# A fused attention and two-layer chain: variances asked for at the normalisation, a new order of gates and loads in the first batch, output products opened in five banks, and two weights merged in three passes

## The reference

```python
kv  = einsum('bhsd,bhse->bhde', k, v);  o = einsum('bhsd,bhde->bhse', q, kv)
x   = o / sqrt(mean(o*o, -1) + 1e-6) * g_norm          # 8 heads of 64
# 4 experts, each a causal attention; the two with the larger gate logits count
q, k, v = x @ wq[e], x @ wk[e], x @ wv[e]
a   = softmax(q @ k.T / 8, causal);   ye = a @ v @ wo[e]
x2  = sum over the two chosen e of softmax weight * ye
# gated layer
h   = gelu(x2 @ w_in);  u, g = h[:, :512], h[:, 512:]
vn  = (g - mean(g)) / sqrt(var(g) + 1e-6) * g_ln
out = x2 + (u * (w_sg @ vn + b_sg)) @ w_out
```

## Time and profile before

| | us |
|---|---|
| median of 3 runs (lowest, highest) | 836.63 (836.17, 839.96) |
| profiled execution, whole | 838.38 |
| its span, first to last instruction | 836.6 |
| PE busy | 812.7 (97%) |
| DVE busy | 484.8 (58%) |
| ACT busy | 370.6 (44%) |
| POOL busy | 193.1 (23%) |

### The profile page before, as it was taken

One profiled execution on the slowest core, in us unless ns is written; L12 is line 12 of the kernel. 1 busy time (PEld: TensorE's weight loads), 2 busy tenths in 40 slices (PEclk: granted clock), 3 DMA queues, 4 the chain that ended last, 5 costly groups with the idle time before them and its releaser, 6 DMA issues.

```text
span 836.6 us, 16871 instructions
## 1 busy us (share of the span) xinstructions
PE 812.7 (97%) x6637; PEld 727.7 (87%) x6637; DVE 484.8 (58%) x1272; ACT 370.6 (44%) x841; POOL 193.1 (23%) x246
## 2 busy tenths in 40 slices
PE   7988999999999999999999999999999999998998
PEld 4787898988889898998989889898989989898896
DVE  1767744485545855478534874458553685548840
ACT  0665513474235632455234661456323563255521
POOL 1621224003320133102230023300332013310320
PEclk9999999999999999999999999999999999999999
DMA  9819005040140304130050400504014000100001
GB/s 268 232 47 220 19 6 122 2 115 1 27 94 2 114 1 78 50 94 22 1 107 14 116 1 16 111 2 114 2 33 89 2 2 1 45 26 2 1 1 63
DMA packets 117406, 47.29 MB, mean 57 GB/s; under 512 B 94352, under 2 KB 110736, under 8 KB 117328
## 3 DMA queue, kind: packets, MB, share of 16 engines
q1 hardware_dynamic: 117328, 46.21, 22.0%
HBM read 35.19 MB, written 9.44 MB: 53 GB/s over the span
## 4 chain that ended last, share of the span: by engine, by line
PE 84%; DVE 10%; ACT 2%; DMA 1%; issue 1%; POOL 0%; SPq 0%; DVEq 0%; ACTq 0%; POOLq 0%
PE w L1025 29%; PE t L1025 23%; PE t L1086 7%; PE w L1056 6%; PE t L1071 5%; PE t L1168 3%; PE t L1153 2%; PE t L1176 2%; PE w L1123 2%; PE w L1235 2%; PE w L1071 2%; DVE bn L839 2%; DVE staged L849 1%; DVE big L834 1%; DVE big L854 1%
## 5 line engine op out<-in xcount | busy, mean ns | idle before, releaser
L1025 PE MATMUL w<-wout_s,big 128*128 128x512 f32 x432 | 108.1, 399 | 1.5 <-DVE big L854 0.6
L1025 PE MATMUL t<-big,wqk_s 128*128 128x288 f32 x768 | 105.7, 296 | 2.3 <-DVE wsgT_s L909 2.3
L1025 PE MATMUL w<-wsgT_s,big 128*128 128x288 f32 x768 | 107.3, 295 | 0.0
L1025 PEld LDWEIGHTS t<-big,wqk_s 128*128 128x128 f32 x768 | 102.5, 188 | 2.7 <-issue 2.6
L1025 PEld LDWEIGHTS w<-wsgT_s,big 128*128 128x128 f32 x768 | 103.8, 189 | 0.0
L811 DVE CUSTOM_DVE_ANT_0 w<-w,causal 128x64 f32<-128x64 f32 (+4 forms) x160 | 74.9, 518 | 38.8 <-PE w L1056 38.1
L1025 PEld LDWEIGHTS w<-wout_s,big 128*128 128x128 f32 x432 | 79.6, 188 | 20.3 <-DVE big L854 3.2
L585 POOL TENSOR_TENSOR yT<-squares,yT 128x256 fp32r<-128x256 f32 (+1 forms) x32 | 22.3, 696 | 283.9 <-ACT yT L710 283.9
L724 ACT ACTIVATE big<-work 128x576 fp32r<-128x576 f32 x32 | 22.0, 686 | 111.5 <-POOL work L612 96.1
L980 DVE SCALAR_TENSOR_TENSOR work<-w,gln_c,bias_t 128x576 f32<-128x576 f32 x32 | 26.2, 818 | 71.7 <-PE w L1025 71.0
L1025 PE MATMUL t<-w_s,yT 128*128 128x512 f32 x240 | 63.2, 404 | 4.5 <-POOL yT L585 4.5
(11 more groups left out here) (122 smaller groups left out, 1418.7 us busy)
## 6 DMA issues: line engine op xcount, KB each, us to landing
kin<-in_k_dram SPq DMA_DIRECT2D x8, 1024.0 KB, 6.3
vin<-in_v_dram SPq DMA_DIRECT2D x8, 1024.0 KB, 9.4
out_dram<-work SPq DMA_DIRECT2D x32, 256.0 KB, 2.1
qin<-in_q_dram SPq DMA_DIRECT2D x112, 72.0 KB, 2.4
staged_win<-in_moe_w_in_dram SPq DMA_DIRECT2D x4, 512.0 KB, 5.3
vin<-in_moe_w_sg_dram SPq DMA_DIRECT2D x4, 288.0 KB, 3.9
kin<-in_k_dram SPq DMA_DIRECT2D x8, 128.0 KB, 2.9
vin<-in_v_dram SPq DMA_DIRECT2D x8, 128.0 KB, 6.6
```

What stands on the lines that cost most here:

```text
L1025: last = nc.tensor.matmul(o, stationary(hs, c), mv(hm, c), start=c == of[0] and p == 0, stop=c == of[-1] and p == len(PASSES) - 1)
```

## The change

1. In part -1 `w2` is made like every other product: `wo` turned and `w_in` are split into HI and LO (unit `win`, ScalarE and VectorE; for `woT` both parts by VectorE) and multiplied in three fp32r passes, pass by pass instead of chunk by chunk. The parts lie in `wsgT_s`, `wout_s` and `wo_s` until these get their own contents.
2. In batch 0 `ranks` stays, the last two `wsgT` units and `qk (0, 1)` come before `weights` and `scale 0`, and `wsgR` before `scale 1`; `qk (1, 1)` takes slot `t0` instead of `t1`.
3. k of batch 1 is loaded as soon as `w_out` is split, v after `wsgT 4` (which is also where GpSimd now clears `vin`), q after `wsgR`.
4. In every batch GpSimd's variance and power stand at `norm j` instead of `h j`, and ScalarE's `vhat` of tiles 3 and 4 after `u 1` and `u 2` instead of `u 0` and `u 1`.
5. In the last batch `scale 2` comes before `values 0`, and `out_y` of all five tiles comes before the first `out_g`, in slots w0, w1, t0, t1, t2.

```diff
-    FIRST = [("woT", 0), ("woT", 1), ("w2", 0), ("w2", 1)] + [("kv", c) for c in range(DC)]
-    FIRST += [("qT", 0), ("qT", 1), ("qT", 2), ("o", 0), ("qT", 3), ("o", 1), ("qT", 4), ("o", 2),
-              ("o", 3), ("w2", 2), ("x", 0), ("o", 4), ("x", 1), ("x", 2), ...
+    FIRST = [("woT", 0), ("woT", 1), ("win", 0), ("win", 1), ("w2", 0), ("w2", 1)] + [("kv", c) for c in range(DC)]
+    FIRST += [("qT", 0), ("qT", 1), ("qT", 2), ("o", 0), ("qT", 3), ("o", 1), ("qT", 4), ("win", 2), ("o", 2),
+              ("o", 3), ("w2", 2), ("x", 0), ("o", 4), ("win", 3), ("x", 1), ("x", 2), ...
...
-        plan += [("ranks", 0), ("g_exp", 0), ("weights", 0), ("qk", (0, 1)), ("scale", 0)] + late(("wsgT", 4))
-        plan += [("qk", (EP, 1)), ("scale", 1)] + late(("wsgR", 0)) + [("qk", (1, 1))] + late(("split", "wo"))
+        if first:
+            plan += [("ranks", 0), ("g_exp", 0), ("wsgT", 3), ("qk", (0, 1)), ("wsgT", 4), ("weights", 0), ("scale", 0), ("qk", (EP, 1)),
+                     ("wsgR", 0), ("qk", (1, 1)), ("scale", 1), ("split", "wo")]
...
-        plan += values(0) + [("scale", 2)] + ([] if last else KV)
+        plan += [("scale", 2)] + values(0) if last else values(0) + [("scale", 2)] + KV
...
-    VHAT_AFTER = {("gelu", 2): 0, ("gelu", 3): 1, ("gelu", 4): 2, ("u", 0): 3, ("u", 1): 4}
+    VHAT_AFTER = {("gelu", 2): 0, ("gelu", 3): 1, ("gelu", 4): 2, ("u", 1): 3, ("u", 2): 4}
...
-    PLAN[B - 1] = attention(False, True) + MLP + [x for x in MIX if x[0] != "turn"] + [x for x in MIXED if x[0] in ("out_y", "out_g")]
+    PLAN[B - 1] = attention(False, True) + MLP + [x for x in MIX if x[0] != "turn"]
+    PLAN[B - 1] += [("out_y", t) for t in range(NT)] + [("out_g", t) for t in range(NT)]
...
             sp.wait_ge(wout_lo, FC)
+            load_kv(1, "k")
+            u.wait_full(sp, 0, ("wsgT", NT - 1))
+            sp.wait_ge(vin_padded, 1)
+            load_kv(1, "v")
             u.wait_full(sp, 0, ("wsgR", 0))
-            sp.wait_ge(vin_padded, 1)
-            load_kv(1)
             load_q_blocks(1)
...
-                    elif kind == "h":
+                    elif kind == "norm":
 
                         pool.wait_ge(var_ready, count(part, NT, j + 1))
...
+                    elif kind == "win":
+                        dve.wait_ge(win_hi, j + 1)
+                        nc.vector.tensor_tensor(win_split[j][:, LO, :], win_st[j], as_f32(win_split[j][:, HI, :]),
+                                                ALU.subtract).then_inc(win_lo, 1)
...
+                        for p, (hs, hm) in enumerate(((HI, HI), (LO, HI), (HI, LO))):
+                            if p == 1:
+                                u.wait_drained(pe, part, ("woT", j // 2))
+                            if p == 2:
+                                pe.wait_ge(win_lo, j + 1)
+                            for c in range(EP):
+                                x = ps[u.slot(part, ("w2", c))]
+                                for h in range(2):
+                                    last = nc.tensor.matmul(x[:, FF * h:FF * (h + 1)], woT_split[:, hs, 256 * j + P * c:256 * j + P * (c + 1)],
+                                                            win_split[j][:, hm, FF * h:FF * (h + 1)], start=j == 0 and p == 0,
+                                                            stop=j == DC - 1 and p == 2)
```

More of the change, by code:

```diff
@@ L156, in moe_chain @@
     SLOT_FIRST = {**SLOT, ("v", 1): "t2", ("v", 2): "t0", ("v", 3): "t2", ("wsgT", 0): "t1", ("wsgT", 1): "t3", ("wsgT", 2): "t1",
-                  ("wsgT", 3): "t3", ("wsgT", 4): "t1", ("wsgR", 0): "t3", ("qk", (EP, 1)): "t2", ("qk", (1, 1)): "t1"}
+                  ("wsgT", 3): "t3", ("wsgT", 4): "t1", ("wsgR", 0): "t3", ("qk", (EP, 1)): "t2", ("qk", (1, 1)): "t0"}
     SLOT_LAST = {**SLOT, ("v", 4): "t3"}
@@ L195, in units @@
                     got.append((("y", j // 2), Y_SLOT[j // 2]))
-            elif kind in ("split", "double", "exp", "scale", "gelu", "wout", "w2e", "yhi", "turn", "T_copy", "y_mul", "ranks",
+            elif kind in ("split", "double", "exp", "scale", "gelu", "wout", "w2e", "yhi", "turn", "T_copy", "y_mul", "ranks", "win",
                           "g_exp", "weights", "norm"):
@@ L207, in units @@
                     got.append((("u", 0), WIDE[0]))
-            elif kind in ("u", "vs", "woT"):
+            elif kind in ("u", "vs"):
                 got.append(((kind, j), WIDE[j % 2]))
             elif kind == "out_y":
-                got.append((("out", j), WIDE[(j - first_out(part)) % 2]))
+                got.append((("out", j), (WIDE + NARROW)[j] if part == B - 1 else WIDE[(j - first_out(part)) % 2]))
             elif kind == "out_g":
@@ L317, in moe_chain @@
         w_hi = sem("w_hi")
+        win_hi = sem("win_hi")
+        win_lo = sem("win_lo")
+        woT_hi = sem("woT_hi")
         wqk_lo = [sem("wqk_lo_0"), sem("wqk_lo_1")]
@@ L379, in moe_chain @@
         win_st = [staged_win[:, r, c * 2 * FF:(c + 1) * 2 * FF] for r in range(2) for c in range(2)]
-        woT_st = [staged_win[:, r, 4 * FF + 256 * c:4 * FF + 256 * (c + 1)] for r in range(2) for c in range(2)]
+        win_split = [wsgT_s[:, :, :, :].rearrange("p s t n -> p s (t n)")[:, :, 2 * FF * c:2 * FF * (c + 1)] for c in range(2)]
+        win_split += [wout_s[:, :, :, :].rearrange("p s c n -> p s (c n)")[:, :, 2 * FF * c:2 * FF * (c + 1)] for c in range(2)]
+        woT_split = wo_s[:, :, :, :].rearrange("p s c n -> p s (c n)")
         wqk_st = staged_wqk[:, :].rearrange("p (c w e h) -> p c w e h", c=DC, w=2, e=E)
@@ L422, in _, with load_kv @@
         def _(sp):
-            def load_kv(b):
-                for x, dst, main in ((k, kin, k_main), (v, vin, v_main)):
+            def load_kv(b, among="kv"):
+                for x, dst, main in ((k, kin, k_main), (v, vin, v_main))[among == "v":1 if among == "k" else 2]:
                     sp.dma_start(dst[PAD:P, 4 * D:NT * D].rearrange("p (h d) -> p h d", h=H),
@@ L588, in body @@
                                                 ALU.subtract).then_inc(yT_lo, 1)
-                    elif kind == "wsgR":
+                    elif (kind, j) == ("wsgT", NT - 1):
                         u.wait_full(pool, part, (kind, j))
@@ L1114, in body @@
                     elif kind == "w2":
-                        if j == 0:
-                            u.wait_drained(pe, part, ("woT", 0))
-                            u.wait_drained(pe, part, ("woT", 1))
-                        pe.wait_ge(w_loaded[f"win_{j}"], 16)
-                        for c in range(EP):
-                            x = ps[u.slot(part, ("w2", c))]
-                            for h in range(2):
-                                last = nc.tensor.matmul(x[:, FF * h:FF * (h + 1)], woT_st[j][:, P * c:P * (c + 1)],
-                                                        win_st[j][:, FF * h:FF * (h + 1)], start=j == 0, stop=j == DC - 1)
-                            if j == DC - 1:
-                                finish(last, ("w2", c))
+                        pe.wait_ge(woT_hi, j // 2 + 1)
+                        pe.wait_ge(win_hi, j + 1)
+                        for p, (hs, hm) in enumerate(((HI, HI), (LO, HI), (HI, LO))):
[9 more added lines that the diff above has]
+                                                            stop=j == DC - 1 and p == 2)
+                                if j == DC - 1 and p == 2:
+                                    finish(last, ("w2", c))
                     elif kind == "wsgT":
```

22 lines of the change are left out of this document (16 added, 6 removed).

## The result

| | before | changed |
|---|---|---|
| median of the runs, us | 837.34 (836.17 to 839.96, 4 runs) | 827.94 (826.71 to 832.14, 4 runs) |
| ratio of the two | 1 | 0.9888 (95%: 0.9866 to 0.9910) |
| profiled execution, us | 838.38 | 827.14 |
| its span, us | 836.6 | 825.4 |
| PE busy, us | 812.7 | 806.5 |

The change makes the kernel 1.12% faster, 9.4 us between the medians; 9.6 us and a time of 827.0 us were forecast. (The forecast counts from 836.63 us, the median of three of the four runs before.) The two profiled executions lie 11.2 us apart.

A forecast was written before the change was run, and what follows sets the result against it. TensorE was taken as the bound, busy 812.7 of 836.6 us, leaving its waits, removable matmuls and low-clock stretches. Terms -0.4 - 1.3 - 4.1 - 3.1 - 0.7 = -9.6 us gave a 827.0 us median, range 822.0 to 831.5.

The forecast's parts named there:

- Part -1: Stage making the merged `w2`: first `qk` 1.0 us earlier undisturbed, -0.4 us taken, between -3.2 and +2.3.
- Rival 2: Part -1: VectorE and GpSimd hold each other up at the shared SBUF ports, +2.3 us there; time 829.7, chance 0.15.
- Part 2: Batch 0's gate order: the 2.3 us wait for `wsgT 4` goes, 1.0 us comes back at `wsgR`; -1.3 us.
- Part 3: Loads in batch 0: the 2.87 us wait for batch 1's v and the half-clock `kv` after it go; -4.1 us.
- Part 4: Gated layer, every batch: `yT` wait only widens the gap before `u 2`; `u 3` gains 0.38 us per batch, -3.1 us.
- Rival 1: Steady batches gain all that PE waited, because VectorE's sequence also moves: 4.5 us more, time 822.5, chance 0.12.
- rival 3: Steady gain is nothing: the wait at `u 3` moves to before the `w_sg` product; time 830.1, chance 0.13.
- Part 5: Last batch: `out_y` first covers the gated-product wait, -0.6 us; `scale 2` first mostly moves a wait, -0.1 us.
- Rival 4: Part -1: PE never leaves the low clock, first `qk` 15.9 us late; slower, time 843.3, chance 0.03.

The follow-up runs named there:

- experiment 4: Kernel before with only the last batch's edits (`scale 2` before `values 0`, all `out_y` before `out_g`); ratio 0.9995 to the kernel before.
- experiment 8: Changed kernel with batch 0's old order of gates and old slot; ratio 0.9915 to the kernel before.
- experiment 9: Changed kernel with ScalarE's `vhat` of tile 2 also moved, from after `gelu 4` to after `u 0`; median 821.56 us, ratio 0.9803 to the kernel before.
- experiment 3: Kernel before with only the merged `w2`, made in three fp32r passes; ratio 0.9989 to the kernel before.
- experiment 10: On top of experiment 9, batch 0's `weights 0` and `scale 0` moved behind `wsgR`; ratio 0.9813 to the kernel before.
- experiment 6: Kernel before with only batch 0's new order of gates and the new slot of `qk (1, 1)`, loads as before; ratio 0.9999 to the kernel before.
- experiment 5: Kernel before with only the new places of batch 1's k, v and q loads, old order of gates; ratio 0.9961 to the kernel before.
- experiment 7: Kernel before with batch 0's new loads and new order of gates together; ratio 0.9927 to the kernel before.
- experiment 1: Kernel before with only GpSimd's variance and power moved to `norm` from `h`; ratio 1.0000 to the kernel before.
- experiment 2: Kernel before with only ScalarE's `vhat` of tiles 3 and 4 moved after `u 1` and `u 2`; ratio 0.9970 to the kernel before.
- experiment 11: On top of experiment 9, the last batch's `scale 2` put back behind `values 0`; median 820.04 us, ratio 0.9794 to the kernel before.

## Why the prediction was right, and where it was not

The time came out 0.9 us from the forecast, and each term but one was right by its mechanism and about its size. That the median came so close is luck in part. Between the two profiles the gain is 11.2 us, 1.6 more than forecast, most of it in part -1. The four runs of the changed kernel differ: 826.71 and 827.14 us at a mean granted clock of 1.000, 828.74 at 0.997 and 832.14 at 0.995. A clock below 1 after 15 us was named as a sign of being wrong; the profile has none, but two of the runs must. Where it fell in them no profile shows; the last batch's wait of 2.05 us is the one long enough for it (experiments 4, 8 and 9).

- **Part -1** was the term that was mis-sized: -0.4 taken, -1.8 in the trace, of which 0.3 us are scatter (experiment 3). Its mechanism held: the last scaling was forecast to end at 33.9 and ended at 33.84, and VectorE's first `wqk` piece right behind it, not PE, set the end. Of the signs, the first `qk` at 34.73 lies outside "within 1 us of 36", and the wait for the piece is 0.1 us where 1.1 was placed (0.4 in five other profiles with the merged `w2`). Two steps were off. The cost held against the term, that the new subtractions and the powers delay each other, does not exist: 1.22 us beside powers of 1.65 and 1.64 us. And the piece was taken to need half of 3.27 us; it took 0.87, because GpSimd's pair had begun 0.95 us earlier (32.81) and the piece met only the tail of its first instruction. Those two are the 0.6 us that I gave up for the ports' sake and some 0.7 us of the piece.
- **Rival 2**, the ports, falls for the powers. The Trainium skill, page "SBUF — State Buffer", section "SBUF: two separate sides", has the later of two such instructions blocked until the other ends. The `wqk` pairs agree with it (3.27 and 2.56 us, each beside a GpSimd pair of 2.97, for as many columns as one new subtraction does in 1.2 us alone); the power of 128x8, which reads SBUF too, does not: a subtraction begun 0.39 us into it, and another 0.19 us into it, took no longer. The delay that rival 2 named is real beside GpSimd's long subtractions, only elsewhere: one in batch 0 makes the wait in the profile of experiment 10 and stands in that of 6, and in the changed kernel it is missed by 0.07 us, which the prediction did not work out.
- **Part 2** held: -1.3 forecast, -1.2 seen, with the wait on `wsgR` of 0.86 us where 1.0 was placed. **Part 3** held: -4.1 forecast, -4.3 seen. The two are not independent, as the sum took them: by experiments 5 to 7 some 2.8 us of the pair exists only when both are made (by the three intervals 0.6 to 5.0 us). Part of this is order alone: with the old loads v sets when PE goes on, however early PE comes to it. The rest is the low clock, 1.5 us behind the 2.30 us wait in experiment 5; the prediction tied it only to the wait for v. The sum came out because it was taken with both made.
- **Part 4** held, and experiments 1 and 2 show each half: 0.0 for the variance, -2.5 us (-3.9 to -1.2) for the order, where -3.1 was forecast for both. Rival 1 (all of 4.5 us more) falls, and so does rival 3: no wait stands ahead of the `w_sg` product.
- **Part 5**: -0.7 forecast, -0.8 in the trace, -0.4 (-1.8 to +0.9) by itself. The reading that `scale 2` only moves a wait was right (0.7 and 1.4 became 2.1), but the move had a price that was not seen: it makes one wait long enough for the low clock (experiments 9 and 11: 1.6 us, and the low clock in three of the five profiles with this wait).
- **Rival 4** (never out of the low clock in part -1) did not come: the first 24 matmuls took 7.69 us, where 11 were its mark and 8.4 the forecast's.

## What to carry to other kernels

A wait is worth what the next one behind it leaves: go along the releaser's own queue, and ask whether it depends on the waiting engine at all (here a 4.5 us wait was worth 0.0, and the 1.7 us one beside it 2.5). Read TensorE's gaps on the weight-load rows, which showed 6.8 us where the matmul rows showed 5.1 and 6.6 came back. Before moving an instruction of VectorE, look at what GpSimd has in SBUF at its new time (experiment 10). Where several waits of some 2 us stand close together, remove them together and keep the rest short, since the low clock can stand behind any one of them that is left.
